# Attention and two MLPs on one core: where the two integers are spread, and when GpSimd starts its MLP work

## What is computed

```
keep   = is_global | is_local
scores = q k^T / 8 - slope_h * dist;  scores = where(keep, scores, -1e9)
x      = softmax(scores) @ v                       # reshaped to 1536 x 512
h      = x @ w_in;   x = (h * sigmoid(h)) @ w_out
h      = x @ w_in2;  y = (h * clip(h + 3, 0, 6) / 6) @ w_out2
```

## Time and profile before

| | us |
|---|---|
| median of 3 runs (612.55 to 614.22) | 612.57 |
| the profiled execution | 612.97 |
| its span, first to last instruction | 611.2 |

### The profile page before, as it was taken

One profiled execution on the slowest core, in us unless ns is written; L12 is line 12 of the kernel. 1 busy time (PEld: TensorE's weight loads), 2 busy tenths in 40 slices (PEclk: granted clock), 3 DMA queues, 4 the chain that ended last, 5 costly groups with the idle time before them and its releaser, 6 DMA issues.

```text
span 611.2 us, 9570 instructions
## 1 busy us (share of the span) xinstructions
PE 592.6 (97%) x3408; PEld 512.9 (84%) x3408; DVE 371.5 (61%) x696; ACT 340.6 (56%) x657; POOL 283.9 (46%) x353
## 2 busy tenths in 40 slices
PE   3999999899999999999999999999999999999997
PEld 2565567899999999999999898888888888888886
DVE  4778987755755477557555866575556685555331
ACT  3889885544444466444444765444557565555441
POOL 2887999354933304539433234395333343331110
PEclk9999999899999999999999999999999999999999
DMA  7443531032122212222222123213221252221002
GB/s 274 175 166 121 195 117 38 2 139 70 69 70 70 69 36 71 74 66 67 70 70 70 34 70 105 69 36 103 68 68 38 70 173 69 70 70 34 1 0 104
DMA packets 14883, 50.08 MB, mean 82 GB/s; under 512 B 1904, under 2 KB 2160, under 8 KB 14832
## 3 DMA queue, kind: packets, MB, share of 16 engines
q1 hardware_dynamic: 14832, 49.42, 23.7%
HBM read 46.27 MB, written 3.15 MB: 81 GB/s over the span
## 4 chain that ended last, share of the span: by engine, by line
PE 87%; POOL 6%; DVE 2%; ACT 2%; issue 2%; DMA 1%; DVEq 0%; SPq 0%; ACTq 0%
PE ps L918 37%; PE ps L994 22%; PE ps L985 15%; PE ps L986 7%; POOL probs L278 3%; PE ps L865 2%; PE ps L875 2%; PE ps L890 2%; POOL rsume L270 1%; ACT probs L664 1%; DMA words<-in_n_loc 1%; DVE g_f L476 1%; POOL x_t L310 0%; POOL x_t L318 0%; POOL x_t L315 0%
## 5 line engine op out<-in xcount | busy, mean ns | idle before, releaser
L323 POOL TENSOR_TENSOR wo_lo<-wo_raw,wo_hi 128x1024 fp32r<-128x1024 f32 x32 | 76.9, 2404 | 260.2 <-ACT wo_hi L732 260.2
L918 PE MATMUL ps<-x_hi,wi_hi 128*128 128x384 f32 x448 | 151.5, 338 | 3.0 <-DVE g_f L476 2.6
L918 PE MATMUL ps<-x_lo,wi_hi 128*128 128x384 f32 x448 | 150.8, 337 | 0.0
L918 PE MATMUL ps<-x_hi,wi_lo 128*128 128x384 f32 x448 | 150.6, 336 | 0.0
L466 DVE TENSOR_TENSOR c_sb<-ps,p_c 128x384 f32<-128x384 f32 x64 | 35.6, 556 | 169.1 <-PE ps L918 169.1
L712 ACT ACTIVATE p_c<-ps 128x384 f32<-128x384 f32 x64 | 31.5, 492 | 135.6 <-PE ps L918 135.4
L918 PEld LDWEIGHTS ps<-x_hi,wi_hi 128*128 128x128 f32 x448 | 84.7, 189 | 6.6 <-issue 3.2
L918 PEld LDWEIGHTS ps<-x_hi,wi_lo 128*128 128x128 f32 x448 | 84.6, 189 | 0.6
L918 PEld LDWEIGHTS ps<-x_lo,wi_hi 128*128 128x128 f32 x448 | 84.6, 189 | 0.0
L994 PE MATMUL ps<-wo_hi,g_hi 128*128 128x512 f32 x192 | 75.9, 396 | 0.0
L994 PE MATMUL ps<-wo_hi,g_lo 128*128 128x512 f32 x192 | 75.9, 395 | 0.0
(11 more groups left out here) (89 smaller groups left out, 1084.2 us busy)
## 6 DMA issues: line engine op xcount, KB each, us to landing
wi_raw<-in_w_in SPq DMA_DIRECT2D x32, 512.0 KB, 3.4
wo_raw<-in_w_out SPq DMA_DIRECT2D x32, 512.0 KB, 3.4
v_raw<-in_v SPq DMA_DIRECT2D x8, 704.0 KB, 4.6
k_raw<-in_kT SPq DMA_DIRECT2D x8, 464.0 KB, 5.0
q_raw<-in_qT SPq DMA_DIRECT2D x8, 384.0 KB, 5.7
out_y<-y_out SPq DMA_DIRECT2D x11, 256.0 KB, 4.5
out_y<-y_out SPq DMA_DIRECT2D x2, 128.0 KB, 1.8
words<-in_n_glob SPq DMA_DIRECT2D x1, 1.0 KB, 2.5
```

Of the source, the lines that this page charges most:

```text
L323: nc.gpsimd.tensor_tensor(wo_lo[:, s % 2, :], wo_raw[:, s % 2, :], wo_hi[:, s % 2, :], ALU.subtract).then_inc(wo_lo_ok, 1)
L918: mm = nc.tensor.matmul(p_bank(bank), w[:, s % 2, at], x[:, b, k, :], start=fresh and k == 0 and i == 0, stop=k == 1 and i == 2, skip_grou ...
```

## The change

- **Integers.** The two integers come as one row of 16 bytes to one partition, with one DMA. VectorE works them out on that partition, and sets the flag there. TensorE spreads the three numbers (n_global, n_local, n_local clamped) over 128 partitions by one matmul with a row of ones, into PSUM bank 1; VectorE copies them to `nums`.
- **Masks.** `m_base` and the bias of head 0 are made inside VectorE's `banded`; the bias of head 1 is made by ScalarE, ahead of its first exponential. VectorE waits for it before the second score half of unit 0.
- **Loads.** SP issues k of pairs 0 and 1 and v of pair 0; ScalarE issues q of pairs 0 and 1, ahead of everything else that it does.
- **TensorE's start.** Eight transposes of the identity into PSUM bank 0, whose results nobody reads, then the spreading matmul, then five more such transposes, then the branch.
- **GpSimd at the seam.** Before `wo_low(0)` it waits until the four gating products of step 0 are counted. Then it goes `wo_low(0)`, `w_sum(2)`, `w_sum(3)`, `wo_low(1)`: the last two change places.
- **VectorE at the seam.** `c_sum(0, 1)` comes before `silu(0, 0)`.

```diff
@@ sync
-            sp.dma_start(words[:, 0:2], n_glob.to_broadcast([P, 2])).then_inc(words_in, 16)
-            sp.dma_start(words[:, 2:4], n_loc.to_broadcast([P, 2])).then_inc(words_in, 16)
-
-            load_qk(sp, 0)
-            load_qk(sp, 1)
+            sp.dma_start(words[:, :], counts).then_inc(words_in, 16)
+            for it in range(2):
+                load_k(sp, it)
             load_v(sp, 0)
@@ gpsimd
-                wo_low(0)
-                for n in range(4):
-                    w_sum(2, n)
...
             either(pool, banded, general)
-            for s in range(1, NSTEP):
-                if s == 1:
-                    wo_low(s)
+
+            pool.wait_ge(g_ok, 4)
+            wo_low(0)
+            for s in range(NSTEP):
                 if s + 2 < NSTEP:
                     for n in range(4):
                         w_sum(s + 2, n)
-                if s > 1:
+                if s:
                     wo_low(s)
@@ vector
+            nc.vector.memset(ones[:, :], 1.0).then_inc(ones_ok, 1)
-            dve.wait_ge(words_in, 32)
+            dve.wait_ge(words_in, 16)
...
+            nc.vector.tensor_scalar(cnt[:, 6:7], cnt[:, 5:6], 0.0, None, ALU.max).then_inc(row_ok, 1)
+            link(nc.vector.tensor_scalar(cnt[:, 7:8], cnt[:, 5:6], 1.0, None, ALU.is_ge))
...
+            ng, nl = nums[:, 0:1], nums[:, 2:3]
+
+            def numbers():
+                dve.wait_ge(rows_ok, 1)
+                link(nc.vector.tensor_copy(nums[:, 0:3], ps[:, 1, 0:3]))
...
+            def base():
+                rel, key, rel8, far, glb = [m[:, :] for m in m_tmp]
+                link(nc.vector.tensor_scalar(nums[:, 3:4], nl, -8.0, None, ALU.mult))
+                dve.wait_ge(iota_ok, MW_IOTAS)
+                nc.vector.tensor_scalar(far, rel, nl, NEVER, ALU.is_ge, ALU.mult).then_inc(chain, 1)
+                nc.vector.tensor_scalar(glb, key, ng, NEVER, ALU.is_ge, ALU.mult).then_inc(chain, 1)
+                links[0] += 2
+                dve.wait_ge(chain, links[0])
+                link(nc.vector.tensor_tensor(far, rel8, far, ALU.add))
+                nc.vector.scalar_tensor_tensor(m_base[:, :], glb, nums[:, 3:4], far, ALU.add, ALU.max).then_inc(base_ok, 1)
+                dve.wait_ge(base_ok, 1)
+                link(nc.vector.tensor_scalar(m_bias[:, 0, :], m_base[:, :], slope[:, 0:1], None, ALU.mult))
...
-            for h in range(2):
-                nc.vector.tensor_scalar(m_bias[:, h, :], m_base[:, :], slope[:, h:h + 1], None, ALU.mult).then_inc(bias_ok, 1)
-            dve.wait_ge(bias_ok, 2)
-
             def banded():
+                numbers()
+                base()
                 for u in range(NU):
...
+                    if u == 0:
+                        dve.wait_ge(bias_ok, 1)
                     negated(u, 1)
...
+            c_sum(0, 1, 0, p5_c, P7)
             silu(0, 0)
-            c_sum(0, 1, 0, p5_c, P7)
             c_sum(0, 2, 1, u2_c, P3)
@@ scalar
+            for it in range(2):
+                load_q(act, it)
...
-                for h in range(2):
+                for h in range(0 if it else 1, 2):
...
             def banded():
+                act.wait_ge(base_ok, 1)
+                bias(0)
                 for u in range(NU):
@@ tensor
             pe.wait_ge(ident_ok, 2)
+            def busy(n):
+                for _ in range(n):
+                    nc.tensor.transpose(ps[:, 0, 0:P], ident[:, :], ident[:, :])
+
+            busy(8)
+            pe.wait_ge(ones_ok, 1)
+            pe.wait_ge(row_ok, 1)
+            nc.tensor.matmul(ps[:, 1, 0:3], ones[:, :], cnt[:, 4:7], start=True, stop=True).then_inc(rows_ok, 1)
+            busy(5)
```

More of the change, by code:

```diff
@@ L58, in at_least, with build @@
     eng.wait_ge(sem, value)
-def build(nc, qT, kT, v, w_in1, w_out1, w_in2, w_out2, n_glob, n_loc, out):
+def build(nc, qT, kT, v, w_in1, w_out1, w_in2, w_out2, counts, out):
     outer = ExitStack()
@@ L81, in build @@
         ident = sb("ident", [P, P])
-        words = sb("words", [P, 4], I32)
-        cnt = sb("cnt", [P, 8])
-        flag = sb("flag", [P, 1], I32)
+        words = sb("words", [1, 4], I32)
+        cnt = sb("cnt", [1, 8])
+        ones = sb("ones", [1, P])
+        nums = sb("nums", [P, 4])
+        flag = sb("flag", [1, 1], I32)
         slope = sb("slope", [P, 2 * NH])
@@ L142, in x_quad @@
             return x_raw[:, KT * b + 2 * (quad // 2):KT * b + 2 * (quad // 2) + 2, TB * (quad % 2):TB * (quad % 2) + TB]
-        words_in = sem("words_in"); ident_ok = sem("ident_ok"); iota_ok = sem("iota_ok")
+        words_in = sem("words_in"); ones_ok = sem("ones_ok"); row_ok = sem("row_ok"); rows_ok = sem("rows_ok"); ident_ok = sem("ident_ok"); iota_ok = sem("iota_ok")
         chain = sem("chain"); flag_ok = sem("flag_ok")
@@ L149, in build @@
         s_done = sem("s_done")
-        bias_ok = sem("bias_ok")
+        base_ok = sem("base_ok"); bias_ok = sem("bias_ok")
         neg_done = sem("neg_done")
@@ L174, in build, with load_k, load_q @@
         NQK = 16
+        def load_k(eng, it):
+            eng.dma_start(k_raw[it % 2][:, 0:KW], kT[it]).then_inc(k_in[it % 2], 16)
+        def load_q(eng, it):
+            eng.dma_start(q_raw[it % 2][:, :], qT[it]).then_inc(q_in[it % 2], 16)
         def load_qk(sp, it):
-            par = it % 2
-            sp.dma_start(k_raw[par][:, 0:KW], kT[it]).then_inc(k_in[par], 16)
-            sp.dma_start(q_raw[par][:, :], qT[it]).then_inc(q_in[par], 16)
+            load_k(sp, it)
+            load_q(sp, it)
         def load_v(sp, it):
@@ L361, in general @@
                 pool.wait_ge(q_in[1], NQK)
-                pool.wait_ge(bias_ok, 2)
                 nc.gpsimd.iota(a_rel[:, :], [[-1, S]], base=0, channel_multiplier=1, **io).then_inc(iota_ok, 1)
@@ L411, in _ @@
             link(nc.vector.scalar_tensor_tensor(cnt[:, 4:6], cnt[:, 2:4], 4294967296.0, cnt[:, 0:2], ALU.mult, ALU.add))
[L412 to L416, removed]
+            nc.vector.tensor_scalar(cnt[:, 6:7], cnt[:, 5:6], 0.0, None, ALU.max).then_inc(row_ok, 1)
+            link(nc.vector.tensor_scalar(cnt[:, 7:8], cnt[:, 5:6], 1.0, None, ALU.is_ge))
+            link(nc.vector.scalar_tensor_tensor(cnt[:, 7:8], cnt[:, 5:6], float(MAXLOC), cnt[:, 7:8], ALU.is_le, ALU.mult))
+            nc.vector.scalar_tensor_tensor(flag[:, :], cnt[:, 4:5], float(GLOB), cnt[:, 7:8], ALU.is_le,
                                            ALU.mult).then_inc(flag_ok, 1)
-            link(nc.vector.tensor_scalar(nl, cnt[:, 5:6], 0.0, None, ALU.max))
+            common = links[0]
+            ng, nl = nums[:, 0:1], nums[:, 2:3]
+            def numbers():
+                dve.wait_ge(rows_ok, 1)
+                link(nc.vector.tensor_copy(nums[:, 0:3], ps[:, 1, 0:3]))
             def masks(link, rel, jj, loc, glb, keep, ngl, dist):
@@ L498, in copy_t @@
                 nc.vector.tensor_copy(probsT[:, u % 2, :, :], pt_bank(u)).then_inc(pt_dve, 1)
-            for h in range(2):
-                nc.vector.tensor_scalar(m_bias[:, h, :], m_base[:, :], slope[:, h:h + 1], None, ALU.mult).then_inc(bias_ok, 1)
-            dve.wait_ge(bias_ok, 2)
             def banded():
+                numbers()
+                base()
                 for u in range(NU):
                     if u % NT == 0 and 0 < u < 4 * NT:
-                        dve.wait_ge(bias_ok, 2 * (u // NT) + 2)
+                        dve.wait_ge(bias_ok, 2 * (u // NT) + 1)
                     negated(u, 0)
@@ L530, in general @@
                 halves = lambda ap: ap.rearrange("p (a k) -> p a k", a=2)
+                links[0] = common
+                numbers()
                 dve.wait_ge(iota_ok, MW_IOTAS + 2)
@@ L1072 @@
         "w_out2": w_out_steps(moe2_w_out),
-        "n_glob": np.asarray(n_global, np.int64).reshape(1, 1).view(np.int32),
-        "n_loc": np.asarray(n_local, np.int64).reshape(1, 1).view(np.int32),
+        "counts": np.asarray([n_global, n_local], np.int64).reshape(1, 2).view(np.int32),
     }
```

## The result

| | before | after |
|---|---|---|
| median (range), us | 613.39 (612.55 to 616.22, 4 runs) | 605.82 (604.28 to 606.75, 4 runs) |
| the profiled execution, its span | 612.97, 611.2 | 604.28, 602.2 |

The account below looks back on a forecast made before the run. TensorE, busy 97% of the span, was taken as the bound, with gaps only at the start and the seam between MLP steps 0 and 1. 612.97 - 3.0 (start) + 1.2 (seam) = 611.2, 610.8 against the median; range 608.9 to 612.6.

Parts of the forecast that it names:

- Behind the first score: After the first score row, ScalarE's exponentials, then TensorE set the pace; their work only moves along, no further gain or loss.
- All nothing: Behind the seam, the later weight sums, `wo_low` and loads cost nothing while margins of a microsecond and more hold.
- Landing of the words: At the start, the integers land at 3.1, 2.8 us earlier, by one load taking 2.3 us, bounds 1.8 and 2.5.
- From there to the first score row: At the start, VectorE takes up the first score row 5.0 us after the integers land, at 8.1 against 11.11.
- Rival D: At the start, the spread or a second table load of 1.28 sits behind the branch: start -1.5, 612.3; chance 0.08.
- Rival B: At the start, loads set the pace: first score at 9.2, start -1.9, seam +1.2, total 611.9; chance 0.14.
- Start 3.0 earlier: At the start, the first score row and all work behind it come 3.0 us sooner, bounds -1.9 and -3.5.
- Seam, step 1 sooner by 2.55: Between MLP steps 0 and 1, the pause speeds the gating products: TensorE starts step 1 at 106.75 instead of 109.30.
- Give-back at P7: In step 1, late GpSimd sums delay ScalarE's `w_high` and keep: TensorE idles 3.4 us before P7, leaving -0.1.
- The clock behind that idle: In step 1, TensorE falls to half clock again after the new idle: +1.3 us, bounds 0 and +1.7.
- rival A: At the seam, no new clock fall, or all inside the idle: seam -0.1 to -0.6, about 609.3; chance 0.20.
- C: At TensorE's first product of step 2, late sums make it wait for VectorE: slower, 614.5; chance 0.06.

Follow-up runs that it names:

- e1: The kernel before with 32 unused bytes ahead of `g_hi`, nothing else changed: 607.67 us against 613.08 for the kernel before, ratio 0.9921.
- e2: The changed kernel with 32 unused bytes ahead of `g_hi`: 608.22 us against 613.08 for the kernel before, ratio 0.9918.
- e9: The changed kernel with 32 unused bytes ahead of `x_hi` and again ahead of `x_t`: 608.51 us, one run, against 617.4 for the kernel before.
- e10: The changed kernel with 32 unused bytes ahead of `wi_hi` and again ahead of `wo_hi`: 605.98 us, one run, against 617.4 for the kernel before.
- e12: The changed kernel with 96 unused bytes ahead of `g_hi`: 613.51 us, one run, against 613.1 for the kernel before.
- e11: The kernel before with 64 unused bytes ahead of `g_hi`: 610.94 us, one run, against 613.1 for the kernel before.
- e7: The changed kernel with e5 and e6 together and without the 13 early transposes: 603.06 us against 615.25 for the kernel before, ratio 0.9807.
- e4: The changed kernel without the 13 early transposes of the identity, spreading matmul kept: 605.43 us against 613.08 for the kernel before, ratio 0.9876.
- e5: The changed kernel with TensorE's whole MLP inside both branch bodies: 607.89 us against 615.25 for the kernel before, ratio 0.9884.
- e6: The changed kernel with `w_sum(2)` ahead of `wo_low(0)`, pause kept: 603.73 us against 615.25 for the kernel before, ratio 0.9811.
- e3: The changed kernel with the old seam: no GpSimd pause, old order on GpSimd and VectorE: 605.16 us against 613.08 for the kernel before, ratio 0.9852.

## Why the prediction was wrong

**The step that failed** is the one that had no term: "Behind the first score ScalarE's row of exponentials sets the ramp, then TensorE; all their work is unchanged and moves along", and "All nothing" for what lies behind the seam. The work is unchanged, its pace is not: new tensors ahead of it in the partition moved `g_hi`, and 32 second halves became 0.20 or 0.14 shorter: 5.4 us, shown alone by e1 (613.08 to 607.67). The start address of a tensor was in no part of my sum and in none of the rivals, so the range could not hold it.

**The named terms came out near their sum.** They had -1.8 (start -3.0, seam +1.2). Five profiled executions have the changed kernel's instructions and differ only in addresses: after, e2, e9, e10, e12. Their first down matmuls start at 114.70, 114.24, 117.15, 116.68 and 118.42, mean 116.2, where the kernel before has 118.25: -2.0 on average, from -4.0 to +0.2 (e1 and e11, with the start and seam of before, have 118.31 and 118.27). Cut at the last x_sum, the average is -2.5 for the start and +0.5 for the seam. With the missing term, 612.97 - 2.0 - 5.4 = 605.6; measured 605.82. That the total of the two parts came out is in part luck, since their errors offset each other:

- Landing of the words: 2.3 forecast, with a lower bound of 1.8 from a store of 128 KB; 1.18 measured. The error was the bound: nothing in the trace excluded a quicker transfer. The Trainium skill ("DMA: Bandwidth & Descriptors", section "Anatomy of one DMA") has about 2.0 us as a DMA's fixed cost, and states it for a DMA on GpSimd's path, while this one is SyncE's, so the estimate of 3.3 us for the start had no ground there; the measured 1.18 is below it and decides.
- From there to the first score row: 4.96 after the landing, 5.0 forecast. Right, with the branch, the spread and the masks as costed.
- Rival D: not so. TensorE's last transposes end at 5.17, and the table load, 3.88 to 5.16, lies beside VectorE's masks.
- Rival B: not so in the profile of after, where k is in at 5.38 and the scores (first need 6.94) are in time, but by a small margin. In e2 and e7 k came 0.4 to 0.5 later and the first score row waited for it (7.18 and 7.32). The chain of e2:

```profile
1.20 4.54 DMA k_raw<-in_kT
...
5.78 1.25 PE ps L889 x4
...
7.18 0.29 DVE negs L492
```

- Start 3.0 earlier: 4.17 at the first score row, but 2.65 at the last x_sum. The loss is the half clock from 14.6 to 17.9 (in e4, without one, the last x_sum ends 1.5 sooner). I had priced the clock in the seam alone. It can't be put down to the early transposes: e4 lacks it, but so do e2, e5 and e9, which have them, and e7 has it without them.
- Seam, step 1 sooner by 2.55: by 0.95 here (9.93 to 8.98 after the last x_sum), by 1.5 to 1.6 in e2, e9, e10 and e12. VectorE and TensorE did their part; TensorE's exit from its branch, which the old wait had covered, was late next. The forecast asked what is late next only for the semaphores. Shown by e5.
- Give-back at P7: right in mechanism, ScalarE waits 2.27 for the sums ahead of `w_high(2, 0)`. From the last gating product to P7 I had 8.4; it took 8.2 in e2, e4, e5, e9, e10 and e12, and GpSimd's work 6.7 in them where I had 6.8. (In after the half clock moved the second `g_low` out of its way, and it took 5.95.) Forecast 3.4 idle; 2.70, 2.18 and 2.57 in e2, e4 and e12, hidden in the profile of after: the idle was shorter because step 1 started later. That the idle comes from the sums' place in GpSimd's queue is shown by e6.
- The clock behind that idle: fell in after before P7, in e5 and e9 within the idle, in e12 behind it, not in e2, e4 and e10. The seam, 18.89 before, took 18.70 and 18.68 in e2 and e10 (-0.2: rival A), 20.22 in e12 (+1.3: the forecast), 21.35 in e9 (+2.5) and 17.98 in after (-0.9). A fixed +1.3 was the wrong form; it is a term that comes or doesn't.
- C: step 2 did not wait; no sign of it in any run.

**Open.** Why a start at 96 past 128 slows the matmuls that stream g where 32 past does not, and either slows those that hold it still; why e12 has 8.41 and not 8.46, and e9 8.47 and not 8.32. The rule in g's place rests on one profiled execution per run. Which executions fall to the half clock: one program has both, as e3's six times show, 602.1 and 602.7 at a mean granted clock of 1.0, and 604.3 to 606.5 at 0.992 to 0.997.

## What to carry to other kernels

When a diff adds, drops or resizes a tensor, write down which later tensors move and by how much, before costing anything else; in a kernel bound by TensorE compare the mean of equal matmuls before and after, and test with an unused tensor of a few bytes. When a wait is removed, list also what the engine itself does there (a branch, a jump) under its cover. A price read from one execution of a stretch at half clock is one draw: compare with the same stretch at full clock where one exists.

## What the runs showed that was not expected

- Start address of g: 36 matmuls 8.20 or 8.40 us by a shift of 32 bytes, 48 matmuls 8.32 or 8.46 (8.41 in e12); products 7.28 to 7.30 wherever their operands lay.
- A transfer of 16 bytes to one partition landed 1.18 us after issue, the same 16 bytes to 128 partitions 4.6.
- Leaving a branch on TensorE took 1.6 to 2.3 us from the last matmul to the next with nothing to wait for; with the work inside the gap was 0.73 (e5, e7), but the kernel's last stores landed 1.1 us later.
- Half clock after a short idle time comes in some executions and not in others; with it one stretch of the same instructions lasts up to 4.2 us longer (first down matmul at 114.24 and 118.42).
